# V's blocks in three transfers, block means moved by ScalarE's transfers, block maxima placed later

## The reference

```
block, window = (32, 16);  nb = S // block              # 24 blocks a head
k_sum = k.reshape(B, H, nb, block, D).max(axis=3)       # block maxima of K
v_sum = v.reshape(B, H, nb, block, D).mean(axis=3)      # block means of V
scores_l = scale * q @ k^T, where |i - j| < window, else -1e9
scores_s = scale * q @ k_sum^T + log(block)
a = softmax([scores_l, scores_s])
x = a @ [v, v_sum]
```

## Time and profile before

| | us |
|---|---|
| median of 3 runs (lowest, highest) | 510.46 (508.37, 512.42) |
| the profiled execution | 508.42 |
| its span | 506.6 |
| PE busy | 486.9 (96%) |
| ACT busy | 212.5 (42%) |
| DVE busy | 230.8 (46%) |
| POOL busy | 133.8 (26%) |

### The profile page before, as it was taken

One profiled execution on the slowest core, in us unless ns is written; L12 is line 12 of the kernel. 1 busy time (PEld: TensorE's weight loads), 2 busy tenths in 40 slices (PEclk: granted clock), 3 DMA queues, 4 the chain that ended last, 5 costly groups with the idle time before them and its releaser, 6 DMA issues.

```text
span 506.6 us, 8571 instructions
## 1 busy us (share of the span) xinstructions
PE 486.9 (96%) x3312; PEld 408.9 (81%) x3312; DVE 230.8 (46%) x623; ACT 212.5 (42%) x433; POOL 133.8 (26%) x130
## 2 busy tenths in 40 slices
PE   4998998999899999999999999999999999999997
PEld 3776776788898998999888888888888888888885
DVE  3476666267726436442664554333332332332331
ACT  2577777347625436443744433232212213212222
POOL 3987969802200020034454543000000000000000
PEclk9999999999999999999999999999999999999999
DMA  9999994710000000440000000020000002000002
GB/s 189 211 224 229 217 215 140 281 52 0 2 0 1 0 1 1 154 180 0 1 0 1 0 1 1 0 84 0 1 0 1 0 0 83 0 0 0 0 0 83
DMA packets 45766, 29.83 MB, mean 59 GB/s; under 512 B 39596, under 2 KB 39596, under 8 KB 44716
## 3 DMA queue, kind: packets, MB, share of 16 engines
q1 hardware_dynamic: 45732, 29.37, 23.0%
HBM read 26.21 MB, written 3.15 MB: 58 GB/s over the span
## 4 chain that ended last, share of the span: by engine, by line
PE 83%; DVE 5%; DMA 3%; POOL 2%; SPq 2%; ACT 2%; issue 2%; DVEq 0%; POOLq 0%; ACTq 0%
PE bank L911 12%; PE bank L913 12%; PE bank L912 11%; PE bank L1122 9%; PE bank L1123 9%; PE bank L1121 9%; PE bank L1077 4%; PE bank L1079 4%; PE bank L1078 4%; DMA vblocks<-in_v 3%; PE bank L991 2%; PE bank L955 2%; PE bank L1063 2%; DVE hx L794 1%; DVE ln L809 1%
## 5 line engine op out<-in xcount | busy, mean ns | idle before, releaser
L669 ACT ACTIVATE ex<-bank 128x512 f32<-128x512 f32 x48 | 28.7, 599 | 127.7 <-PE bank L913 127.7
L913 PE MATMUL bank<-yt_lo,w2in_hi 128*128 (+1 forms) x192 | 74.7, 389 | 0.0
L912 PE MATMUL bank<-yt_hi,w2in_lo 128*128 (+1 forms) x192 | 74.7, 389 | 0.0
L1121 PE MATMUL bank<-w2out_hi,g_hi 128*128 128x512 f32 x192 | 74.7, 389 | 0.0
L1122 PE MATMUL bank<-w2out_lo,g_hi 128*128 128x512 f32 x192 | 74.7, 389 | 0.0
L911 PE MATMUL bank<-yt_hi,w2in_hi 128*128 (+1 forms) x192 | 74.7, 389 | 0.0
L1123 PE MATMUL bank<-w2out_hi,g_lo 128*128 128x512 f32 x192 | 74.7, 389 | 0.0
L889 DVE TENSOR_SCALAR ex<-ex 128x512 f32<-128x512 f32 x48 | 21.6, 451 | 116.3 <-ACT ex L669 116.3
L894 DVE TENSOR_TENSOR g_lo<-gf,g_hi 128x512 fp32r<-128x512 f32 x48 | 46.5, 969 | 36.0 <-ACT g_hi L677 36.0
L677 ACT ACTIVATE g_hi<-gf 128x512 fp32r<-128x512 f32 x48 | 30.4, 634 | 49.0 <-DVE gf L891 49.0
L1077 PE MATMUL bank<-lnt_hi,wout_hi 128*128 128x384 f32 x128 | 45.6, 356 | 1.6 <-DVE lnt_lo L848 1.6
(11 more groups left out here) (103 smaller groups left out, 844.7 us busy)
## 6 DMA issues: line engine op xcount, KB each, us to landing
w2in_raw<-in_w_in SPq DMA_DIRECT2D x1, 4096.0 KB, 12.5
w2out_raw<-in_w_out SPq DMA_DIRECT2D x4, 1024.0 KB, 9.4
vblocks<-in_v SPq DMA_DIRECT2D x15, 256.0 KB, 5.4
kraw<-in_k SPq DMA_DIRECT2D x16, 192.0 KB, 6.3
qraw<-in_q SPq DMA_DIRECT2D x16, 192.0 KB, 5.3
out<-osb SPq DMA_DIRECT2D x12, 256.0 KB, 2.1
vw<-in_v SPq DMA_DIRECT2D x7, 384.0 KB, 6.5
win_raw<-in_w_in SPq DMA_DIRECT2D x4, 512.0 KB, 6.5
```

The costliest lines, as they stand in the source:

```text
L912: pe.matmul(acc, al, bh, start=False, stop=False)
L913: last = pe.matmul(acc, ah, bl, start=False, stop=(i == n - 1))
L1121: pe.matmul(dst, g_hi[:, j % GS, cols], w2out_hi[:, j, :], start=(j == 0), stop=False)
```

## The change

Four edits:

1. Heads 0 and 1 keep their two small loads, now into half 1 of `vblocks`. The blocks of heads 2 to 15 (336 rows of 8 KB) are loaded in CHUNKS = 3 DMAs over 128, 128 and 80 partitions. GpSimd sums three chunks where it summed four.
2. SP's order: chunk 0 stands where the second half of the old chunk 0 stood, chunk 1 moves from before Q of pair 2 to behind V of pair 2, chunk 2 comes behind Q of pair 5.
3. For pairs 1 to 7 GpSimd no longer copies the means into `vw`. `move_means(n)` on ScalarE's queue issues one DMA for each head (two for heads 7 and 12, whose rows lie in two chunks), 16 in all, each of 24 x 12 pieces of 256 B from SBUF to SBUF; `attend` waits for `means_moved[n]`.
4. On VectorE `block_maxima` goes from t = 2 (or 3) to t = 4, behind `low_x`.

```diff
-            def load_vblocks(c, i):
-
-                if c >= 2:
+            def load_vblocks(c):
+
+                if c >= 1:
                     sp.wait_ge(vmean_ready, c)
-                b0 = (HPM * c + i) * NB
...
+                b0 = 2 * NB + c * P
+                sp.dma_start(vblocks[0:chunk_rows(c), c % 2, :], v_blocks[b0:b0 + chunk_rows(c), :]
+                             ).then_inc(vblocks_loaded[c], 16)
...
             load_v(0)
             load_k(1)
-            load_vblocks(0, 2)
-            load_vblocks(0, 3)
+            load_vblocks(0)
             load_q(1)
             load_v(1)
             load_k(2)
-            for i in range(HPM):
-                load_vblocks(1, i)
             load_q(2)
             load_v(2)
+            load_vblocks(1)
             load_k(3)
...
-                if n % 2 == 1 and n // 2 + 1 < MEANS:
-                    for i in range(HPM):
-                        load_vblocks(n // 2 + 1, i)
+                if n == 4:
+                    load_vblocks(2)
...
             def finish_v(n, j0, j1):
                 fill_halo(n, max(j0, 1), j1)
-                spread_means(n, j0, j1)
+                if n == 0:
+                    spread_means(n, j0, j1)
...
+            def move_means(n):
+
+                act.wait_ge(vmean_ready, 2 + pieces_of_means(2 * n + 1)[-1][0])
+                if n >= VS:
+                    act.wait_ge(attn_done, T * (n - VS + 1))
+                for h in range(2):
+                    for c, r0, r1, to in pieces_of_means(2 * n + h):
+                        act.dma_start(vw[LOCAL + to:LOCAL + to + r1 - r0, n % VS, h, :, 0:D],
+                                      vmean[r0:r1, 1 + c, None, :].broadcast_to([r1 - r0, SUBS, D])).then_inc(means_moved[n], 16)
+
+            MOVED_AT = {7: 1, 8: 2, 16: 3, 20: 4, 26: 5, 31: 6, 37: 7}
...
             for u in range(UNITS + X_LAG):
                 n, t = u // T, u % T
+                if u in MOVED_AT:
+                    move_means(MOVED_AT[u])
                 if u < UNITS:
                     exps(u)
...
-                if t == (2 if n else 3) and n + 1 < PAIRS:
-                    block_maxima(n + 1)
                 w = u - X_LAG - 1
                 if w >= 0 and w % TG == TG - 1:
                     low_x(w // TG)
+                if t == 4 and n + 1 < PAIRS:
+                    block_maxima(n + 1)
...
                 if t == 0:
                     pe.wait_ge(halo_filled, n + 2 if n else 1)
-                    pe.wait_ge(means_spread, 2 * n + 4 if n else 2)
+                    if n:
+                        pe.wait_ge(means_moved[n], moves_of_pair(n))
```

More of the change, by code:

```diff
@@ L167, in fused_layers_kernel @@
         first_blocks_loaded = sem("first_blocks_loaded")
-        vblocks_loaded, vsum_step, vmean_ready = [sem("vblocks_loaded0"), sem("vblocks_loaded1")], sem("vsum_step"), sem("vmean_ready")
+        vblocks_loaded = [sem(f"vblocks_loaded{c}") for c in range(CHUNKS)]
+        vsum_step, vmean_ready = sem("vsum_step"), sem("vmean_ready")
+        means_moved = [sem(f"means_moved{n}") for n in range(PAIRS)]
         zeros_ready, consts_ready = sem("zeros_ready"), sem("consts_ready")
@@ L254, in fused_layers_kernel, with chunk_rows, pieces_of_means, moves_of_pair @@
         QUAD, FIRST = P // HPM, 4
+        def chunk_rows(c):
+            return min(P, (B * H - 2) * NB - c * P)
+        def pieces_of_means(head):
+            r0, r1 = (head - 2) * NB, (head - 1) * NB
+            return [(c, max(r0 - c * P, 0), min(r1 - c * P, P), max(c * P - r0, 0))
+                    for c in range(CHUNKS) if r0 < (c + 1) * P and r1 > c * P]
+        def moves_of_pair(n):
+            return 16 * sum(len(pieces_of_means(2 * n + h)) for h in range(2))
         def v_landed(n):
@@ L307, in load_v, with load_first_blocks @@
                                  ).then_inc(v_loaded[s], 16)
-            def load_vblocks(c, i):
-                if c >= 2:
+            def load_first_blocks(i):
+                sp.dma_start(vblocks[i * QUAD:(i + 1) * QUAD, 1, :], v_blocks[i * NB:i * NB + QUAD, :]
+                             ).then_inc(first_blocks_loaded, 16)
+            def load_vblocks(c):
+                if c >= 1:
                     sp.wait_ge(vmean_ready, c)
-                b0 = (HPM * c + i) * NB
-                b1 = min(b0 + QUAD, B * H * NB)
-                loaded = first_blocks_loaded if c == 0 and i < 2 else vblocks_loaded[c % 2]
-                sp.dma_start(vblocks[i * QUAD:i * QUAD + b1 - b0, c % 2, :], v_blocks[b0:b1, :]).then_inc(loaded, 16)
+                b0 = 2 * NB + c * P
+                sp.dma_start(vblocks[0:chunk_rows(c), c % 2, :], v_blocks[b0:b0 + chunk_rows(c), :]
+                             ).then_inc(vblocks_loaded[c], 16)
             def load_win(i):
@@ L327, in _ @@
             load_q(0)
[L328 to L329 removed]
+            load_first_blocks(0)
+            load_first_blocks(1)
             load_v(0)
             load_k(1)
[L332 to L333 removed]
+            load_vblocks(0)
             load_q(1)
@@ L417, in block_means @@
             def block_means(c):
[L419 to L423, removed]
+                pool.wait_ge(vblocks_loaded[c], 16)
+                rows = slice(0, chunk_rows(c))
                 sum_blocks(vblocks[rows, c % 2, :], BLOCK * D // 2)
-                pool.tensor_scalar(vmean[rows, c, :], vblocks[rows, c % 2, 0:D], 1.0 / BLOCK, None, ALU.mult).then_inc(vmean_ready, 1)
+                pool.tensor_scalar(vmean[rows, 1 + c, :], vblocks[rows, c % 2, 0:D], 1.0 / BLOCK, None, ALU.mult).then_inc(vmean_ready, 1)
                 pool.wait_ge(vmean_ready, c + 2)
@@ L431, in first_means @@
                 rows = slice(0, P // 2)
-                sum_blocks(vblocks[rows, 0, :], BLOCK * D // 8)
-                pool.tensor_scalar(vmean[rows, 0, :], vblocks[rows, 0, 0:D], 1.0 / BLOCK, None, ALU.mult).then_inc(vmean_ready, 1)
+                sum_blocks(vblocks[rows, 1, :], BLOCK * D // 8)
+                pool.tensor_scalar(vmean[rows, 0, :], vblocks[rows, 1, 0:D], 1.0 / BLOCK, None, ALU.mult).then_inc(vmean_ready, 1)
                 pool.wait_ge(vmean_ready, 1)
@@ L486, in _ @@
             finish_v(1, 0, SUBS)
+            finish_v(2, 0, SUBS)
             block_means(1)
-            finish_v(2, 0, SUBS)
             finish_win(0)
+            finish_v(3, 0, SUBS)
             finish_win(1)
-            finish_v(3, 0, SUBS)
-            block_means(2)
             finish_v(4, 0, SUBS)
             finish_win(2)
+            block_means(2)
             finish_v(5, 0, SUBS)
-            block_means(3)
+            finish_win(3)
             finish_v(6, 0, SUBS)
-            finish_win(3)
             finish_v(7, 0, SUBS)
@@ L980, in attend @@
                     pe.wait_ge(halo_filled, n + 2 if n else 1)
-                    pe.wait_ge(means_spread, 2 * n + 4 if n else 2)
+                    if n:
+                        pe.wait_ge(means_moved[n], moves_of_pair(n))
+                    else:
+                        pe.wait_ge(means_spread, 2)
                 if n == 0 and 2 * t == FIRST:
```

12 lines of the change are left out of this document (5 added, 7 removed).

## The result

The changed kernel took 515.30 us (median of 4 runs, 513.03 to 517.73) against 509.50 us for the kernel before, ratio 1.0106 (95% interval 1.0064 to 1.0148): slower by 1.06%. That is inside the range of 507.0 to 517.5, but 4.4 us above the forecast of 510.9, and against a median of before that a fourth execution had brought down by 1.0 us: forecast were +0.4 us, measured +5.8. The profiled execution took 517.73 us (span 515.9), the longest of the four and 9.3 us over that of before, so it shows the loss larger than the median does. Medians in this document are of all executions of a kernel; ratios leave out those in the slower of the two states that a kernel's executions fall into.

A forecast was written before the change was run, and what follows sets the result against it. PE, 83% of the chain of waits, was taken as the bound; only its gaps in the first 100 us count. -4.7 + 0.9 + 2.1 + 1.2 + 0.9 = +0.4 us on the 510.46 median gave 510.9, range 507.0 to 517.5.

The forecast's parts named there:

- Gaps in front of Q: PE's idle time before turning Q closes once block_maxima no longer delays low_x on VectorE: 4.2 us gained over six pairs.
- K of pair 5 without slack: In the attention, K of pair 5 lands at 56.3 while PE wants it at 55.4: 0.9 us lost.
- GpSimd's copy: PE's one wait in front of attend, ended by GpSimd's copy of the means, goes: 0.51 us gained.
- 1 MB in front of Q of pair 1: A 1 MB load replaces 512 KB ahead of Q of pair 1, so PE waits 0.9 us (0 to 1.0).
- ScalarE's issues: DMA issues on ScalarE, 0.5 us each, partly covered by ACTIVATEs, delay exps and copy_pt: 2.1 us lost.
- the prediction's own covers: ScalarE time hiding issues: 1.22 us at t = 2, 0.77 at t = 1, 0.56 at t = 4.
- Means of pair 1 late: Pair 1's moved means land 4 us after the second issue, so PE waits in front of attend: 1.2 us lost.
- The moves' packets: Added 256 B pieces delay loads by 0.3 to 1.04 us a pair, 0.7 taken; first felt at K of pair 5.
- the slower rival: The held issue: ScalarE's issues held like SP's, median 1.26 us, +11 us, 521.5; over 1% slower from 0.9 us. Chance 0.18.
- The forecast's own range: Gaps close and new waits give the gain back: -3 to +3 us, 507.5 to 513.5; chance 0.55.
- no clear change: Whole-kernel outcome between 505.4 and 515.6 us, a change under 1% (5.1 us) either way; chance 0.77.

The follow-up runs named there:

- the run with the maxima alone: The kernel before with only block_maxima moved behind low_x at t = 4: 509.43 us, ratio 1.000.
- the quiet run: The changed kernel, but SP waits for pair 1's moved means before issuing chunk 1 of V's blocks and all that follows: 511.32 us, ratio 1.0038.
- the run with the maxima back: The changed kernel with block_maxima back at t = 2 (t = 3 in pair 0), in front of low_x: 518.96 us, ratio 1.0184 to before.
- the shorter stall: The kernel before with five small ACTIVATEs in front of exps(31), some 2.0 us of ScalarE, no transfer added: 510.35 us, ratio 1.0025.
- late w_in: The kernel before with block_maxima moved and w_in's loads issued two pairs later, GpSimd copying means of pairs 3 to 7 earlier: 508.29 us, ratio 0.9961.
- everything that helped: The changed kernel with pair 1 copied by GpSimd, heads moved singly, w_in late and chunk 0 behind Q of pair 1: 509.43 us, ratio 0.995 to before.

## Why the prediction was right, and where it was not

**Gaps in front of Q, 4.2 us gained:** right in its mechanism. They are gone in every variant with the maxima moved, and back without it. That the gain need not survive was in the forecast as K of pair 5 without slack, and the run with the maxima alone shows that as one of three places where it went. In the changed kernel PE was too late for it: K of pair 5 did not wait, so the term of 0.9 us was 0.

**GpSimd's copy, 0.5 us gained:** its wait is gone.

**1 MB in front of Q of pair 1, 0.9 us:** 0 in the changed kernel's profile, 0.4 to 0.9 in the four variants with the same loads, 1.7 and 2.0 in the two that load it in two transfers. The step was sound, the size varies from one execution to the next. What the prediction did not have is that such a wait can prolong the slow matmuls of the start.

**ScalarE's issues, 2.1 us:** the mis-sized term. The step took 0.5 us an issue; measured 0.8, and 1.4 for two of the 16, and 5.25 us on the path in the profiled execution. The places were right: nothing at t = 2 (1.22 us of cover was put down, and two issues are 1.6, the rest is slack that I had not counted), everything at t = 1 and t = 4. With the measured lengths the prediction's own covers give 1.5 + 1.8 + 2.1 + 0.8 = 6.2 us. Left out of it was that a move also waits for GpSimd's means in ScalarE's order.

**Means of pair 1 late, 1.2 us:** right in place, wrong in size, 4.18 us. I took 4 us to landing because ScalarE's own queue is empty. An empty queue was no help: the transfers already out come first, and 8.9 us passed. The sentence that gave the high end (6.3 us to landing, 3.5 us of waiting) was nearer.

**The moves' packets, 0.3 to 1.04 us a pair:** no wait for K or Q in the changed kernel's profile after 20 us bears on it; open. The rule of the Trainium skill that issuing engines are not separate DMA queues ("DMA: Bandwidth & Descriptors", section "Issuing engines are not separate DMA queues") was weighed only for these packets' cost, and the trace bears on it where it mattered, in the latency of the first urgent transfer. That both queues share the engines agrees with the quiet run. That their transfers interleave shows only from 28 us on (491 pieces beside 1130); in the 4.4 us before, 8 pieces moved.

**Missing altogether:** the clock. No term stood for it, and in the profiled execution it cost 5.2 us, as much as the issues.

The sum of +0.4 us should have read, with these sizes, 4.18 + 5.25 - 4.7 = +4.7 before the clock, and the median came out 5.8 us above that of before.

So there is luck in the number. Four of the sum's terms were off: two of 0.9 us came out at nothing, 2.1 and 1.2 were 5.25 and 4.18, and the clock had none. The forecast's own range, 507.5 to 513.5, was missed. The measured 515.30 lies in the stated range only because that was widened by half of the slower rival. That rival, the held issue, had the right sign. It was to decide from 0.9 us an issue, and 14 of the 16 stayed under that; the first, long in every run, is not held by SP. But 0.8 us was nearly enough: the 16 issues took 13.9 us, and by the rival's own sum 13.9 - 6.5 - 2.6 = +4.8. And slower by 1.06% is just past the 1% that divided two of the outcomes; I had given the side of "no clear change" 0.77 and the slower one 0.18.

## What to carry to other kernels

A transfer on an otherwise empty queue was not quick here, when another queue had filled the engines: count its landing from what is already out, and don't put on that path a result that a compute engine can copy in 1.7 us. An issue on ScalarE costs it 0.8 us here; it is free only beside an instruction of that length, with nobody waiting for the next one. What the issue waits for, ScalarE waits for too, and everything behind it in its order (1.3 us here). Where a gap is closed, look at which load and which copy were just on time: the gain goes there, and only with these moved as well does it show (0.9961, against 1.000 and 1.0013 alone). And look at the clock of every execution before a difference of 0.5% is put down to an edit.

## What the runs showed of the hardware

- The first DMA issue on ScalarE took 1.41 us, later ones 0.8 (1413 and 795 ns in the changed kernel, 1.41 and 0.80 with SP's queue quiet), three of them 1.03 to 1.47; SP's shortest took 0.43.
- Two transfers of 72 KB on ScalarE's empty queue had landed 10.4 us behind the start of the first issue (8.9 behind the second's) with SP's loads out, with 8 pieces moved in the first 4.4 us, and within 4.6 us (3.1) without them; on GpSimd's queue they took 7.3 and 8.4 us.
- Behind 20 us PE ran at the lower clock for 3 to 16 us behind waits of 1.30 (the run with the maxima back), 1.44 (the shorter stall's profile, at 23.44), 1.45 (quiet), 1.53, 1.62 (late w_in), 1.77, 1.79, 2.18, 2.74, 3.2 and 7.23 us. It kept the clock behind 1.44 (quiet, at 70.89), 1.62 ("issue", everything that helped, at 76.61) and 1.70 us, and behind all shorter than 1.3. So the length of the wait alone doesn't decide; what does stays open.
- In every profile the matmuls are slow at first, until 16 to 22 us (29 in the two with waits of 1.7 and 2.0 us for Q of pair 1), while the clock column reads 1.00: there the durations tell more than the column.
- PE stopped inside a group of matmuls without a wait in the program, mostly at two places: in front of the fourth matmul of `ks,qt` (0.61, 1.16 and 2.74 us in three runs) and in front of the third of `vw,pt` (0.80, 0.85 and 1.62 us in three others). The profiles of the kernel before and of the changed one show neither; the cause is open.
